# Reissuing the loads of an attention fill, moving constant rows to GpSimd, and halving ScalarE's high-part copies in a fused attention and two-MoE kernel

## The chip, the cores and the metric

The kernel runs on one NeuronCore of a Trainium2 chip. TensorE (PE, with its weight loads PEld), VectorE (DVE), ScalarE (ACT), GpSimd (POOL) and SyncE (SP) each run their own instruction stream and meet at semaphores. Times are microseconds on the device; the metric is the median over several runs.

## What is computed

A causal attention over 2 batches, 8 heads, 576 tokens and head size 64, whose scores carry a bias from a running sum; its output feeds a top-2 mixture of 8 experts, and that feeds a second mixture in which all 8 experts take every token. Everything is float32.

```python
# attention (B, H, S, D = 2, 8, 576, 64)
scores = q @ k.T / sqrt(D)
cum = cumsum(maximum(s, 0))
bias = -(cum[..., :, None] - cum[..., None, :])
scores = where(causal, -1e9, scores + minimum(bias, 0))
x = softmax(scores) @ v                      # -> (1152, 512)
# first mixture: gate with noise, the two best experts of 8
x = sum_k top2_w[k] * relu(x @ w1[e_k]) @ w2[e_k]
# second mixture: 8 rounds of row and column balancing of exp(logits), all experts
out = sum_e P[:, e] * (relu(x @ w1b[e]) @ w2b[e])
```

## The kernel before

The matmuls take float32 operands split into a high and a low part: ScalarE rounds to the high part, another engine subtracts for the low part, and PE adds the products up. The program has three stages: attention (8 heads), the sparse experts, the dense experts. The change touches the attention stage alone.

Attention works through 80 steps `k`, ten to a head (`HEAD`), five to a unit (`STEPS`, one batch of one head). Every engine has its own loop over `k` and runs parts of later steps ahead. PE does in step `k`: `rough(k + 13)` (rough scores of one query tile, for the row maximum), `turn_max` (turning two rows of maxima), `scores(k + 4)` and `mix(k)` (probabilities times values, with 65 columns a matmul). DVE does `row_max(k + 13)`, and after each unit `finish` (L1098 writes the unit's output to `x_sb`). ACT does `place_max` and `exponentials(k + 4)`, and between them the high parts of a coming head: `high_k(h)` at `k + 18 = 10 h` and `high_q(h)` at `k + 17 = 10 h`, each one copy. POOL cuts the diagonal of the probabilities (`cut`) and makes the low parts of a coming head in 8 pieces (`low_part`, from `k = 10 h - 14`; semaphore `low`).

PE waits in `rough(0)` of a head for `q_high`, `k_doubled`, `cum_loaded` and `q_rows_ready`. `scores` of a head waits for all its low pieces. `rough(k)` waits for `row_max(k - 2)`.

SP issues all loads in one order written out by hand. For a head these are `load_raw` (three transfers of 288 KB: keys, queries, keys again), `load_cum` (two rows each of the high and the low part of the running sum, put into rows 64 and 65 of `k_top`, one row of one batch at a time: four transfers of 2.25 KB), `load_v` (two transfers), `double_k` and `double_q` (the high parts copied to other partitions). Ring buffers hold 2 raw heads, 3 heads of `k_top`, `k_two`, `q_top`, `v`, and 2 heads of `q_two`. `load_raw(h)` may start when the low pieces of head `h - 2` are done:

```python
for h in range(2, H):
    sp.wait_ge(low, LOWS * (h - 1))
    load_raw(h)
    ...load_cum(h), load_v(h), double_k(h)...
    sp.wait_ge(scores_ready, HEAD * (h - Q_RING + 1))
    double_q(h)
    ...one 512 KB piece of the first expert's weights, for h = 3 to 6...
```

Before the first step PE runs `WARM_UPS` matmuls on constants (`keep_warm`, two passes each), and one half as wide between the rough steps up to `k = -5`. What stands before `k = -4`, when the first `scores` are issued, is called the fill here. In the fill, DVE clears rows 64 to 127 of the three `q_top` buffers and puts ones into rows 64 and 65 (`q_rows(w)`, two memsets each; the tiles `q_top` and `k_two` lie inside `w2l` and `w2h`, and the rows of the trace bear those names), and POOL puts ones into the same rows of `k_top`.

Of the kernel before, what the change touches and what calls it, by code (L numbers as in the profile page):

```python
# [15 lines left out]
P = 128  # L16
# [11 lines left out]
def build(nc, qT, kT, v_rows, v_tail, s, wg, wn, noise, w1, w2, gate2, w1b, w2b, out, cum_dram, x_dram, y_dram):  # L28
# [21 lines left out]
    with ExitStack() as ctx:  # L50
# [99 lines left out]
        cum_high = sem("cum_high")  # L150
        cum_low = sem("cum_low")
# [117 lines left out]
        WARM_UPS = 6  # L269
# [3 lines left out]
        K_HIGH_AHEAD, Q_HIGH_AHEAD, LOW_AHEAD = 18, 17, 14  # L273
# [48 lines left out]
        def _(sp):  # L322
            sp.dma_start(cum_s[0:G, :], s).then_inc(s_loaded, 16)

            def load_raw(h):
# [31 lines left out]
            load_cum(0)  # L357
            load_raw(1)
            double_q(0)
            load_v(0)  # L360
            load_cum(1)
            load_cum(2)
            double_k(1)
            load_v(1)
            double_q(1)
            load_v(2)
            for h in range(2, H):
                sp.wait_ge(low, LOWS * (h - 1))
                load_raw(h)
# [9 lines left out]
                double_k(h)  # L379
                sp.wait_ge(scores_ready, HEAD * (h - Q_RING + 1))  # L380
# [61 lines left out]
        def _(pool):  # L442
# [54 lines left out]
            for k in range(-LOW_AHEAD, ALL):  # L497
                if k >= 0:
# [60 lines left out]
        def _(pe):  # L559

            def rough(k):
                h, b, t = head_of(k), half_of(k), rough_tile(k)
                w, rows, width = h % HEADS_RING, rows_in(t), min(S, (t + 1) * P)
                if k % HEAD == 0:
# [280 lines left out]
        def _(act):  # L845
# [22 lines left out]
            def high_k(h):  # L868
                w = h % RAW_RING
# [4 lines left out]
                act.copy(k_two[h % HEADS_RING], k_raw[:, w, :]).then_inc(k_high, 1)  # L874

            def high_q(h):
                w = h % RAW_RING
# [563 lines left out]
```

## Time and profile before

| | us |
|---|---|
| median of 3 runs | 1310.83 |
| the three runs | 1299.89, 1310.83, 1320.83 |
| the profiled execution's own time | 1305.9 |
| its span in the trace | 1303.9 |
| PE busy | 1257.8 (96% of the span) |

PE's busy time is modelled: matmuls overlap, and a full share doesn't tell how fast they go. The granted clock (PEclk) does: 1.00 stands for 2.4 GHz and 0.50 for 1.2 GHz. Attention takes the first 169 us of the span, the sparse experts and the dense experts the rest.

### The profile page before, as it was taken

The page shows a single profiled execution, that of the slowest core. Times are in us where ns is not written, and L with a number is a line of the kernel's source. Part 1 is how long each engine was busy: PE and PEld are TensorE (multiplying, and loading weights), DVE is VectorE, ACT ScalarE, POOL GpSimd, SP SyncE. Part 2 cuts the span into 40 slices and gives each one's busy share as a digit, 9 for nine tenths or more (in the row PEclk, how much of TensorE's full clock was granted, in tenths as well). Part 3 has the DMA queues.
Part 4 walks back from the last instruction along what each step waited for, and adds up shares of the span by engine and source line. Part 5 has one row for each costly group of instructions (what it writes and reads, how often), then busy time and mean ns, then how long its engine had stood idle before and what let it go on. Part 6 is the DMA issues. An engine that isn't in the chain of part 4 may idle for free.

```text
span 1303.9 us, 17447 instructions
## 1 busy us (share of the span) xinstructions
PE 1257.8 (96%) x6607; PEld 1118.2 (86%) x6607; DVE 489.6 (38%) x1095; ACT 362.7 (28%) x682; POOL 146.5 (11%) x221
## 2 busy tenths in 40 slices
PE   7999948999999979999999999999999999999999
PEld 5888837888888857999999999999999999999997
DVE  6333457455554443344224214214214214313321
ACT  3434624344444423123113113112112112112211
POOL 5434621111110252000000000000000000000000
PEclk8556977999999979999999999999999999999999
DMA  6434253344454653001101101101101101100000
GB/s 138 107 92 116 46 205 111 125 170 171 171 175 170 202 178 129 1 1 65 65 1 64 64 0 64 64 0 64 64 0 64 64 0 64 64 0 0 24 24 24
DMA packets 24757, 102.90 MB, mean 79 GB/s; under 512 B 5440, under 2 KB 10048, under 8 KB 20752
## 3 DMA queue, kind: packets, MB, share of 16 engines
q1 hardware_dynamic: 18288, 85.89, 19.8%
q0 software_dynamic: 3360, 11.01, 2.9%
q10 hardware_dynamic: 3072, 5.51, 1.2%
q8 instruction: 22, 0.36, 0.1%
q14 instruction: 15, 0.12, 0.0%
HBM read 87.68 MB, written 10.22 MB: 75 GB/s over the span
## 4 chain that ended last, share of the span: by engine, by line
PE 90%; DVE 3%; DMA 2%; POOL 1%; SPq 1%; issue 1%; ACT 1%; DVEq 0%; POOLq 0%; ACTq 0%
PE bank L700 14%; PE bank L699 14%; PE bank L698 13%; PE bank L680 13%; PE bank L681 13%; PE bank L682 13%; PE bank L630 4%; PE bank L579 2%; PE bank L613 1%; PE bank L614 1%; DMA k_raw<-in_kT 1%; PE bank L732 1%; POOL w1l L493 1%; DMA x_sb<-x_dram,gather_at 1%; SPq L344 1%
## 5 line engine op out<-in xcount | busy, mean ns | idle before, releaser
L680 PE MATMUL bank<-xTh,w1h 128*128 128x384 f32 (+1 forms) x1024 | 343.7, 336 | 3.0 <-DVE xTl L1141 1.6
L681 PE MATMUL bank<-xTl,w1h 128*128 128x384 f32 (+1 forms) x1024 | 341.7, 334 | 0.0
L682 PE MATMUL bank<-xTh,w1l 128*128 128x384 f32 (+1 forms) x1024 | 341.2, 333 | 0.0
L937 ACT ACTIVATE hh<-bank 128x384 fp32r<-128x384 f32 (+1 forms) x256 | 123.4, 482 | 656.6 <-PE bank L682 654.8
L700 PE MATMUL bank<-w2h,hl 128*128 128x512 f32 (+1 forms) x768 | 303.6, 395 | 0.0
L699 PE MATMUL bank<-w2l,hh 128*128 128x512 f32 (+1 forms) x768 | 302.1, 393 | 0.0
L698 PE MATMUL bank<-w2h,hh 128*128 128x512 f32 (+1 forms) x768 | 301.0, 392 | 0.0
L1161 DVE SCALAR_TENSOR_TENSOR hl<-bank,hh 128x384 fp32r<-128x384 f32 (+1 forms) x256 | 139.4, 544 | 371.4 <-ACT hh L937 367.8
L680 PEld LDWEIGHTS bank<-xTh,w1h 128*128 128x128 f32 x1024 | 193.5, 189 | 5.5 <-issue 2.0
L681 PEld LDWEIGHTS bank<-xTl,w1h 128*128 128x128 f32 x1024 | 193.4, 189 | 1.2
L682 PEld LDWEIGHTS bank<-xTh,w1l 128*128 128x128 f32 x1024 | 193.3, 189 | 0.0
L699 PEld LDWEIGHTS bank<-w2l,hh 128*128 128x128 f32 (+1 forms) x768 | 142.3, 185 | 34.7
L698 PEld LDWEIGHTS bank<-w2h,hh 128*128 128x128 f32 (+1 forms) x768 | 142.5, 185 | 33.2
L700 PEld LDWEIGHTS bank<-w2h,hl 128*128 128x128 f32 (+1 forms) x768 | 142.6, 186 | 32.6
L1188 DVE SCALAR_TENSOR_TENSOR x_sb<-bank,share_now,x_sb 128x512 f32<-128x512 f32 x63 | 47.2, 750 | 259.5 <-PE bank L700 259.5
L1165 DVE TENSOR_TENSOR w2l<-raw,w2h 128x512 fp32r<-128x512 f32 x120 | 82.9, 690 | 0.0
L630 PEld LDWEIGHTS bank<-v_sb,probT 128*128 128x128 f32 (+1 forms) x480 | 74.5, 229 | 6.1 <-issue 1.2
L941 ACT CAST w2h<-raw 128x512 fp32r<-128x512 f32 x128 | 78.3, 612 | 0.0
L630 PE MATMUL bank<-v_sb,probT 128*128 128x65 f32 (+1 forms) x480 | 75.8, 310 | 0.4 <-POOL probT L487 0.4
L1079 DVE CUSTOM_DVE_ANT_0 unused<-bank,causal 64x576 fp32r<-64x576 f32 (+4 forms) x80 | 43.0, 541 | 80.0 <-PE bank L579 79.5
L1107 DVE TENSOR_TENSOR w1l<-raw,w1h 128x1024 fp32r<-128x1024 f32 x60 | 69.5, 1220 | 2.9 <-ACT w1h L916 2.9
L916 ACT CAST w1h<-raw 128x1024 fp32r<-128x1024 f32 x60 | 58.5, 1059 | 0.0
(171 smaller groups left out, 719.7 us busy)
## 6 DMA issues: line engine op xcount, KB each, us to landing
raw<-in_w SPq DMA_DIRECT2D x15, 2048.0 KB, 7.9
raw<-in_w1b SPq DMA_DIRECT2D x8, 2048.0 KB, 7.7
raw<-in_w2b SPq DMA_DIRECT2D x8, 2048.0 KB, 7.8
k_raw<-in_kT SPq DMA_DIRECT2D x16, 288.0 KB, 5.9
y_dram<-x_sb ACTq DMA_DIRECT2D x16, 256.0 KB, 3.0
q_raw<-in_qT SPq DMA_DIRECT2D x8, 288.0 KB, 5.6
q_two<-w2l SPq DMA_DIRECT2D x8, 288.0 KB, 3.2
x_dram<-x_sb SPq DMA_DIRECT2D x1, 2304.0 KB, 9.3
```

What stands on the lines that cost most here:

```text
L630: mm = pe.matmul(bank[rows, OUT_AT + n % 2, t * (HD + 1):(t + 1) * (HD + 1)], probT[:, n % UNIT_RING, at:at + nrow], v_sb[:, w, j, (HD + 1 ...
L680: pe.matmul(dst, w1h[:, c, fs], xTh[:, c, ts], start=(c == 0), stop=False)
L681: pe.matmul(dst, w1h[:, c, fs], xTl[:, c, ts], start=False, stop=False)
L682: mm = pe.matmul(dst, w1l[:, c, fs], xTh[:, c, ts], start=False, stop=(c == DC - 1))
L698: pe.matmul(dst, hh[:, f, ts], w2h[:, f, :], start=(f == 0), stop=False)
L699: pe.matmul(dst, hh[:, f, ts], w2l[:, f, :], start=False, stop=False)
L700: mm = pe.matmul(dst, hl[:, f, ts], w2h[:, f, :], start=False, stop=(f == FC - 1))
L937: act.activation(hh[:, f, 0:n_cols], bank[:, f % UP_BANKS, 0:n_cols], ACT.Relu).then_inc(st.hh_ready, 1)
L941: act.copy(w2h[:, f, :], raw2[:, f, :]).then_inc(st.w2h_ready, 1)
L1107: v.tensor_tensor(w1l[:, c, :], raw1[:, c, :], w1h[:, c, :].bitcast(F32), ALU.subtract).then_inc(st.w1_ready, 1)
L1161: v.scalar_tensor_tensor(out=hl[:, f, 0:n_cols], in0=bank[:, f % UP_BANKS, 0:n_cols], scalar=0.0, in1=hh[:, f, 0:n_cols].bitcast(F32), op0 ...
L1165: v.tensor_tensor(w2l[:, f, :], raw2[:, f, :], w2h[:, f, :].bitcast(F32), ALU.subtract).then_inc(st.w2_ready, 1)
```

## The change

- **SP's order in the fill.** The raw loads of heads 0 and 1 are issued first. Of head 0 the four rows of the running sum are then loaded one by one (batch 0 first). The high and low running sums of all heads are stored to a piece of DRAM (`cum_rows`, inside `x_dram`, which is not yet in use), and from head 1 on `load_cum` is one transfer from there. In the fill that makes 27 transfers instead of 31 (the raw load of head 2 counted in both), and one instead of four for each later head's sums.
- **SP's order in the loop.** `load_raw(h + 1)` comes right behind `double_k(h)`, ahead of the wait of `double_q(h)` and of the weights' piece.
- **Waits of PE.** `rough(0)` waits for batch 0's two rows alone (`cum_first`); batch 1's are waited for five steps later.
- **Constant rows.** POOL clears and sets the rows of `q_top` as well as those of `k_top` (`constant_rows`): those of buffers 0 and 1 at the start, those of buffer 2 behind the low pieces of head 0. DVE no longer does.
- **High parts.** ScalarE's copies are made in halves of 576 columns (1024 columns of the weights in halves of 512), one half behind each of four successive `exponentials`, from `k + 19 = 10 h`.
- **Warm-ups.** 8 instead of 6.

```diff
-        WARM_UPS = 6
+        WARM_UPS = 8
...
-        K_HIGH_AHEAD, Q_HIGH_AHEAD, LOW_AHEAD = 18, 17, 14
+        HIGH_AHEAD, LOW_AHEAD = 19, 14
...
         def high_at(k):
-            kh, qh = divmod(k + K_HIGH_AHEAD, HEAD), divmod(k + Q_HIGH_AHEAD, HEAD)
-            return (kh[0] if kh[1] == 0 else None, qh[0] if qh[1] == 0 else None)
+            h, part = divmod(k + HIGH_AHEAD, HEAD)
+            return (h, *divmod(part, 2)) if h > 1 and part < 4 else None
...
+            cum_rows = x_dram[0:2 * H * N // DM].rearrange("a (c d) -> (a c) d", d=P).rearrange("(g x) d -> g (x d)", g=G).rearrange(
+                "g (r s) -> g r s", r=2)
...
             def load_cum(h):
                 w = h % HEADS_RING
                 if h < HEADS_RING:
                     sp.wait_ge(aug_ready, 2 + h)
-                for row, part, ready in ((HD, cum_h, cum_high), (HD + 1, cum_l, cum_low)):
-                    if h == 0:
-                        sp.wait_ge(ready, 1)
-                    for b in range(B):
-                        sp.dma_start(k_top[w][row:row + 1, b * S:(b + 1) * S].bitcast(F32),
-                                     part[h * B + b:h * B + b + 1, :].bitcast(F32)).then_inc(cum_loaded[w], 16)
+                if h == 1:
+                    sp.wait_ge(cum_stored, 32)
+                sp.dma_start(k_top[w][HD:HD + 2, :].rearrange("r (b s) -> r b s", b=B).bitcast(F32),
+                             cum_rows[h * B:(h + 1) * B].rearrange("b r s -> r b s")).then_inc(cum_loaded[w], 16)
...
             load_raw(0)
-            load_cum(0)
             load_raw(1)
+            sp.wait_ge(aug_ready, 2)
+            sp.wait_ge(cum_high, 1)
+            first_cum(HD, cum_h, 0, cum_first)
+            sp.wait_ge(cum_low, 1)
+            first_cum(HD + 1, cum_l, 0, cum_first)
+            first_cum(HD, cum_h, 1, cum_loaded[0])
+            first_cum(HD + 1, cum_l, 1, cum_loaded[0])
             double_q(0)
+            sp.dma_start(cum_rows[:, 0, :], cum_h[0:G, :].bitcast(F32)).then_inc(cum_stored, 16)
+            sp.dma_start(cum_rows[:, 1, :], cum_l[0:G, :].bitcast(F32)).then_inc(cum_stored, 16)
+            double_k(1)
+            load_cum(1)
             load_v(0)
-            load_cum(1)
+            sp.wait_ge(low, LOWS)
+            load_raw(2)
+            double_q(1)
             load_cum(2)
-            double_k(1)
             load_v(1)
-            double_q(1)
             load_v(2)
             for h in range(2, H):
-                sp.wait_ge(low, LOWS * (h - 1))
-                load_raw(h)
...
                 double_k(h)
+                if h + 1 < H:
+                    sp.wait_ge(low, LOWS * h)
+                    load_raw(h + 1)
                 sp.wait_ge(scores_ready, HEAD * (h - Q_RING + 1))
                 double_q(h)
...
-            for w in range(HEADS_RING):
+            def constant_rows(w):
                 pool.memset(k_top[w][HD:P, :].bitcast(F32), 1.0).then_inc(aug_ready, 1)
-            pool.wait_ge(aug_ready, HEADS_RING + 1)
+                pool.memset(q_top[w][HD:P, :].bitcast(F32), 0.0).then_inc(q_rows_clear, 1)
+                pool.wait_ge(q_rows_clear, w + 1)
+                pool.memset(q_top[w][HD:HD + 2, :].bitcast(F32), 1.0).then_inc(q_rows_ready, 1)
+            constant_rows(0)
+            constant_rows(1)
...
             for k in range(-LOW_AHEAD, ALL):
+                if k == LOWS - LOW_AHEAD:
+                    pool.wait_ge(low, LOWS)
+                    constant_rows(2)
+                    pool.wait_ge(q_rows_ready, 3)
...
-                    pe.wait_ge(cum_loaded[w], 64 * (h // HEADS_RING) + 64)
+                    if h == 0:
+                        pe.wait_ge(cum_first, 32)
+                if h == 0 and k == STEPS:
+                    pe.wait_ge(cum_loaded[0], 32)
+                elif h and k % HEAD == 0:
+                    pe.wait_ge(cum_loaded[w], 16 * (h // HEADS_RING + (1 if w else 2)))
...
-                act.copy(k_two[h % HEADS_RING], k_raw[:, w, :]).then_inc(k_high, 1)
+                part = act.copy(k_two[h % HEADS_RING][:, cols], k_raw[:, w, cols])
+                if half:
+                    part.then_inc(k_high, 1)
```

On SP, from the first load of the running sum to the raw load of head 2 (`k_raw` and `q_raw` from `in_kT` and `in_qT` are raw loads; `w2l` and `w2h` as sources are the high parts), before:

```order
L344 DMA k_top<-cum_h 1x16x36 [waits cum_high,aug_ready]
...
L333 DMA v_sb<-in_v_rows 128x4x128
L334 DMA v_sb<-in_v_tail 64x128
L344 DMA k_top<-cum_h 1x16x36 [waits aug_ready]
...
L350 DMA k_top<-w2h 64x1152 [waits k_high]
L333 DMA v_sb<-in_v_rows 128x4x128
L334 DMA v_sb<-in_v_tail 64x128
L354 DMA q_two<-w2l 64x1152 [waits q_high]
L333 DMA v_sb<-in_v_rows 128x4x128
L334 DMA v_sb<-in_v_tail 64x128
L327 DMA k_raw<-in_kT 64x1152 [waits low]
```

and now:

```order
L351 DMA k_top<-cum_h 1x16x36 [waits cum_high,aug_ready]
...
L360 DMA q_two<-w2l 64x1152 [waits q_high]
L372 DMA x_dram<-cum_h 16x576
L373 DMA x_dram<-cum_l 16x576
L356 DMA k_top<-w2h 64x1152 [waits k_high]
L347 DMA k_top<-x_dram 2x2x576 [waits cum_stored,aug_ready]
L338 DMA v_sb<-in_v_rows 128x4x128
L339 DMA v_sb<-in_v_tail 64x128
L332 DMA k_raw<-in_kT 64x1152 [waits low]
```

The raw load of head 2 was the 29th transfer of the queue and is the 19th.

On DVE, from its first instruction to the first row maximum (`L1079`, now `L1111`), before:

```order
L1052 MEMSET zeros_g 16x576
L1048 MEMSET w2l 64x1152
L1050 MEMSET w2l 2x1152
L1055 TENSOR_SCALAR cum_p<-cum_s 16x576
L1056 SCALAR_TENSOR_TENSOR cum_s<-cum_p,zeros_g 16x576
L1058 CAST k_top<-k_raw 64x1152
L1060 TENSOR_TENSOR cum_l<-cum_s,cum_h 16x576
L1048 MEMSET w2l 64x1152
...
L1048 MEMSET w2l 64x1152
L1050 MEMSET w2l 2x1152
L1067 COPY rinv<-ones 128x10
L1079 ISA unused,aug<-bank,causal 64x576
```

and now:

```order
L1087 MEMSET zeros_g 16x576
L1088 MEMSET probT 64x2x64
L1089 MEMSET v_sb 64x3x128
L1091 TENSOR_SCALAR cum_p<-cum_s 16x576
L1092 SCALAR_TENSOR_TENSOR cum_s<-cum_p,zeros_g 16x576
L1094 CAST k_top<-k_raw 64x1152
L1096 TENSOR_TENSOR cum_l<-cum_s,cum_h 16x576
L1099 COPY rinv<-ones 128x10
L1111 ISA unused,aug<-bank,causal 64x576
```

The six memsets of `q_top` (under the name `w2l`) are gone from DVE's queue.

On ACT, around the high parts of head 2, before:

```order
L866 CAST w2l<-bank 2x192 [waits max_turned]
L855 ACTIVATE probT<-bank 128x512 [waits scores_ready]
L874 CAST w2h<-k_raw 128x1152 [waits k_again0,k_loaded0]
L855 ACTIVATE probT<-bank 128x448 [waits scores_ready]
L881 CAST w2l<-q_raw 64x1152 [waits q_loaded0]
```

and now:

```order
L900 CAST w2l<-bank 2x192 [waits max_turned]
L889 ACTIVATE probT<-bank 128x512 [waits scores_ready]
L908 CAST w2h<-k_raw 128x576 [waits k_again0,k_loaded0]
L889 ACTIVATE probT<-bank 128x448 [waits scores_ready]
L908 CAST w2h<-k_raw 128x576 [waits k_again0,k_loaded0]
L889 ACTIVATE probT<-bank 128x320 [waits scores_ready]
L917 CAST w2l<-q_raw 64x576 [waits q_loaded0]
```

The wait for the raw keys stands behind the same exponential as before; the second half of the keys and the queries stand one exponential further back.

## Rows read from the trace of the kernel before

**Rows 1.** Windows: busy us of each engine, then PEclk, DMA share, GB/s.

```profile
14.00:15.00 1.00, 0.00 (x0) 0.00 (x0) 0.93 (x3) 0.00 (x0) 0.92 (x2) 0.97 0.98 221
21.00:22.00 1.00, 1.00 (x5) 0.83 (x3) 0.32 (x3) 0.00 (x0) 1.00 (x2) 0.62 0.72 152
35.00:36.00 1.00, 1.00 (x9) 0.78 (x9) 0.90 (x6) 0.84 (x4) 0.46 (x1) 0.71 0.47 97
40.00:60.00 20.00, 20.00 (x95) 17.70 (x96) 6.61 (x28) 6.99 (x17) 6.08 (x13) 0.50 0.23 54
120.00:121.00 1.00, 1.00 (x7) 0.96 (x7) 0.24 (x2) 0.61 (x2) 0.00 (x1) 0.63 0.00 0
```

**Rows 2.** Timeline, 25 to 34 us: start, duration, instruction, idle before and its releaser.

```profile
25.82 0.60 SPq L329 DMA_DIRECT2D k_raw<-in_kT  x1
...
31.84 1.15 ACT L874 CAST w2h<-k_raw 128x1152 fp32r<-128x1152 f32 x1 [2.95 <-DMA k_raw<-in_kT]
...
33.49 0.36 PE L613 MATMUL bank<-w2l,k_top 128*128 128x192 f32 x1 [1.64 <-ACT probT L855]
```

**Rows 3.** Line L1098 on DVE, once in each unit: start and duration.

```profile
35.85 0.42 DVE L1098 TENSOR_TENSOR x_sb<-bank,rinv 128x256 f32<-128x256 f32 x1
...
116.64 0.42 DVE L1098 TENSOR_TENSOR x_sb<-bank,rinv 128x256 f32<-128x256 f32 x1
125.20 0.42 DVE L1098 TENSOR_TENSOR x_sb<-bank,rinv 128x256 f32<-128x256 f32 x1
131.68 0.42 DVE L1098 TENSOR_TENSOR x_sb<-bank,rinv 128x256 f32<-128x256 f32 x1
138.94 0.42 DVE L1098 TENSOR_TENSOR x_sb<-bank,rinv 128x256 f32<-128x256 f32 x1
145.55 0.42 DVE L1098 TENSOR_TENSOR x_sb<-bank,rinv 128x256 f32<-128x256 f32 x1
```

**Rows 4.** Timeline of the fill, 0 to 24 us.

```profile
2.42 8.23 PE L636 MATMUL bank<-causal,ones 128*128 128x512 f32 x12 [2.42 <-POOL causal L452]
2.42 3.05 POOL L456 MEMSET k_top<- 64x1152 f32 x3
...
7.20 0.67 ACT L890 CAST cum_h<-cum_s 16x576 fp32r<-16x576 f32 x1 [4.75 <-DVE cum_s L1056]
...
9.07 3.04 POOL L477 TENSOR_TENSOR q_two<-q_raw,w2l 64x288 fp32r<-64x288 f32 x4 [3.60 <-ACT w2l L881]
...
9.20 0.19 PEld L636 LDWEIGHTS bank<-causal,ones 128*128 128x128 f32 x1 [0.24 <-issue]
...
9.63 0.19 PEld L636 LDWEIGHTS bank<-causal,ones 128*128 128x128 f32 x1 [0.24 <-issue]
...
11.84 0.45 PE L579 MATMUL bank<-k_top,w2l 96*64 96x512 f32 x2 [1.20 <-DMA k_top<-cum_l]
...
12.25 3.39 POOL L477 TENSOR_TENSOR w2h<-k_raw,w2h 64x288 fp32r<-64x288 f32 x4
...
13.33 1.02 DVE L1050 MEMSET w2l<- 2x1152 f32 x1 [0.30 <-PE bank L579]
...
15.65 0.69 PE L579 MATMUL bank<-k_top,w2l 96*128 96x384 f32 x1 [2.19 <-DVE aug L1079]
...
21.87 0.53 PE L579 MATMUL bank<-k_top,w2l 96*128 96x384 f32 x1
...
23.92 0.50 PE L613 MATMUL bank<-w2l,k_top 128*128 128x512 f32 x1
```

**Rows 5.** Timeline around the raw load of head 7, 127 to 137 us.

```profile
127.27 0.60 SPq L329 DMA_DIRECT2D k_raw<-in_kT  x1
...
136.57 0.36 PE L613 MATMUL bank<-w2l,k_top 128*128 128x192 f32 x1 [0.83 <-ACT probT L855]
```

**Rows 6.** DMA issues of the whole run: count, KB each, median us to landing.

```profile
k_raw<-in_kT SPq DMA_DIRECT2D x16, 288.0 KB, 5.9
...
y_dram<-x_sb ACTq DMA_DIRECT2D x8, 160.0 KB, 2.0
```

More of the change, by code:

```diff
@@ L150, in build @@
         cum_high = sem("cum_high")
+        cum_first = sem("cum_first")
+        cum_stored = sem("cum_stored")
         cum_low = sem("cum_low")
@@ L339, in load_cum, with first_cum @@
                     sp.wait_ge(aug_ready, 2 + h)
-                for row, part, ready in ((HD, cum_h, cum_high), (HD + 1, cum_l, cum_low)):
-                    if h == 0:
-                        sp.wait_ge(ready, 1)
-                    for b in range(B):
-                        sp.dma_start(k_top[w][row:row + 1, b * S:(b + 1) * S].bitcast(F32),
-                                     part[h * B + b:h * B + b + 1, :].bitcast(F32)).then_inc(cum_loaded[w], 16)
+                if h == 1:
+                    sp.wait_ge(cum_stored, 32)
+                sp.dma_start(k_top[w][HD:HD + 2, :].rearrange("r (b s) -> r b s", b=B).bitcast(F32),
+                             cum_rows[h * B:(h + 1) * B].rearrange("b r s -> r b s")).then_inc(cum_loaded[w], 16)
+            def first_cum(row, part, b, done):
+                sp.dma_start(k_top[0][row:row + 1, b * S:(b + 1) * S].bitcast(F32), part[b:b + 1, :].bitcast(F32)).then_inc(done, 16)
             def double_k(h):
@@ L866, in place_max, with high_k @@
                 act.copy(q_top[w][ROWS_ROUGH:ROWS_ROUGH + 2, b * S + i0:b * S + i1], bank[0:2, MAX_AT, 0:i1 - i0]).then_inc(max_placed, 1)
-            def high_k(h):
-                w = h % RAW_RING
+            def high_k(h, half):
+                w, cols = h % RAW_RING, slice(half * S, (half + 1) * S)
                 act.wait_ge(k_loaded[w], 16 * (h // RAW_RING) + 16)
@@ L873, in high_k, with high_q @@
                     act.wait_ge(scores_ready, HEAD * (h - HEADS_RING + 1))
-                act.copy(k_two[h % HEADS_RING], k_raw[:, w, :]).then_inc(k_high, 1)
-            def high_q(h):
-                w = h % RAW_RING
+                part = act.copy(k_two[h % HEADS_RING][:, cols], k_raw[:, w, cols])
+                if half:
+                    part.then_inc(k_high, 1)
+            def high_q(h, half):
+                w, cols = h % RAW_RING, slice(half * S, (half + 1) * S)
                 act.wait_ge(q_loaded[w], 16 * (h // RAW_RING) + 16)
@@ L880, in high_q, with high_w1 @@
                     act.wait_ge(scores_ready, HEAD * (h - HEADS_RING + 1))
-                act.copy(q_top[h % HEADS_RING][0:HD, :], q_raw[:, w, :]).then_inc(q_high, 1)
-            def high_w1(c):
+                part = act.copy(q_top[h % HEADS_RING][0:HD, cols], q_raw[:, w, cols])
+                if half:
+                    part.then_inc(q_high, 1)
+            def high_w1(c, half):
+                cols = slice(half * F // 2, (half + 1) * F // 2)
                 act.wait_ge(first_w1[c] if c < DC - 1 else SP_.raw1_loaded, 16)
-                act.copy(w1h[:, c, :], raw1[:, c, :]).then_inc(SP_.w1h_ready, 1)
+                part = act.copy(w1h[:, c, cols], raw1[:, c, cols])
+                if half:
+                    part.then_inc(SP_.w1h_ready, 1)
             act.wait_ge(const_ready, 5)
@@ L890, in _ @@
             act.copy(cum_h[0:G, :], cum_s[0:G, :]).then_inc(cum_high, 1)
-            high_q(0)
-            high_k(0)
-            high_k(1)
-            high_q(1)
-            for k in range(-ROUGH_AHEAD, ALL):
-                kh, qh = high_at(k)
-                if kh is not None and kh > 1:
-                    if kh < H:
-                        high_k(kh)
-                    else:
-                        high_w1(2 * (kh - H))
-                if qh is not None and qh > 1:
-                    if qh < H:
-                        high_q(qh)
-                    else:
-                        high_w1(2 * (qh - H) + 1)
+            for h in range(2):
+                for half in range(B):
+                    high_q(h, half)
+                for half in range(B):
+                    high_k(h, half)
+            for k in range(-ROUGH_AHEAD, ALL):
                 for n, part in turns_at(k):
@@ L911, in _ @@
                     exponentials(k + SCORES_AHEAD)
+                high = high_at(k)
+                if high is not None:
+                    h, of, half = high
+                    if h >= H:
+                        high_w1(2 * (h - H) + of, half)
+                    elif of == 0:
+                        high_k(h, half)
+                    else:
+                        high_q(h, half)
             def split_w1(st, n):
```

13 lines of the change are left out of this document (4 added, 9 removed).

## The prediction, as it was put on record

> **What bounds the kernel now.** I read the stretches with their granted clock first, then the timeline where that clock changes, then the period of a unit. Over the whole run PE is the bound, so in attention, too, the question is what PE waits for and how fast it goes. The second is the larger one. In the stretch from 40 to 60 us PE is busy for 20.00 of 20 us, yet its clock is granted at 0.50, that is 1.2 GHz [rows 1]. The clock has fallen inside the slice from 35 to 36 us (mean 0.71) and is back inside the one from 120 to 121 us (mean 0.63) [rows 1]: 85 us of attention run at the lower level. What PE did just before it fell stands in the timeline: it stood still for 1.64 us up to 33.49, waiting for an exponential, and ScalarE was late with that because its high-part copy of head 2 had waited 2.95 us for the raw keys, whose last transfer SP had issued only at 25.82 [rows 2]. The same pair, a stop and a fall, stands in the fill: 2.19 us of idle up to 15.65 [rows 4], the fall at the end of the slice from 14 to 15, the return inside the slice from 21 to 22 [rows 1]. Shorter stops didn't bring it down: 1.20 us up to 11.84 [rows 4] and 0.83 us up to 136.57 [rows 5].
>
> What the clock costs is read from DVE's one instruction per unit. Seven units between 35.85 and 116.64 took 80.8 us, 11.54 each; after the return, the two without a stall took 6.48 and 6.61, mean 6.55 [rows 3].
>
> **The fill.** PE's two added warm-ups are four passes. At the pace that the last passes had (9.20 to 9.63, 0.43 us), they add 1.7 us to the end at 10.65, so PE reaches `rough(0)` at 12.4; before, it started at 11.84, when the running sum's rows landed [rows 4]. They should now land earlier: DVE starts the sum's chain behind fewer memsets, and two rows instead of four are waited for. They queue behind head 1's raw loads, however. So the warm-ups set the start, at a cost of 0.5 us. The next wait goes away. PE idled from 13.46 to 15.65 for DVE's first row maximum, which stood behind two pairs of memsets of 1.02 us each (the last at 13.33) [rows 4]; they leave DVE's queue. `rough(2)` then follows 1.6 us behind `rough(0)`, as 13.46 does on 11.84: at 14.0 instead of 15.65, a gain of 1.65. From there to the first scores there were five rough steps in 6.2 us, most of them at the low clock, and three in 2.05 us at the high one (21.87 to 23.92) [rows 4], so 1.24 us a step against 0.68. At the high clock DVE's row maxima begin to hold PE, so I take 0.95, the middle; five steps gain 1.45. The fill gains **3.1 us** (between 1.2, if the clock still falls, and 4.4, if 0.68 holds for all), and the first scores start at 20.8 instead of 23.92.
>
> What GpSimd takes over is 2 memsets more per buffer, 1.02 us each by its own three (3.05) [rows 4]. Those of the first two buffers end about 9 us, and it waited for `q_high` until 9.07 in any case [rows 4]; those of the third start behind head 0's low pieces, which end at 15.64, and delay head 1's low pieces by 3.1 us at most. The first reader of these is `scores(10)`, ten steps behind the first scores, past 30 us: nothing. Without that cover it would be 3.1 us. The new wait of SP is the one for `cum_stored`. The two stores are issued at about 10 us; the nearest prices are 2.0 us for a store of 160 KB and 5.9 us for a load in a full queue [rows 6], so it ends between 12 and 16 us. Behind it stand the sum's rows and the values of head 0 and the raw load of head 2, and this last waits for the low pieces until 15.64 anyway. Nothing, or 0.5 us at worst.
>
> **The stall of head 2.** Its raw load was the 29th transfer of SP and is the 19th. It can be issued at 15.7, its last transfer at 17.5, and lands 5.9 us later [rows 6], at 23.4. ScalarE wants it behind the same exponential as before. That was 28.89 (31.84 less 2.95), 5.0 us after the first scores, so now 25.8: 2.4 us to spare. The idle **1.6 us** goes, and with it what preceded the fall of the clock.
>
> **The clock.** If it stays at 2.4 GHz, seven units of 11.54 become seven of 6.55, 34.9 us less, and the unit in which it rose (116.64 to 125.20, 8.56) gives 2.0: **36.9 us**. It needs later raw loads in time at the faster pace. The one load that the trace shows at that pace, of head 7, came too late: the unit took 7.26 instead of 6.55 [rows 3], PE idle 0.83 [rows 5]. In the new order a raw load is released two steps earlier (2.6 us at 1.31 a step) and goes ahead of a 512 KB weight piece instead of behind it. Against a stop of 0.83 that is cover enough, and it gives **0.7 us**.
>
> The Trainium skill speaks against this term. Its page "TensorE: Matmul & The Clock Gate", section "A second HAM failure mode: psum-queue depth-cycling", tells of a kernel in which frequent short idle spells between groups of matmuls swung the clock between its levels, with no long wait. By that the slow stretch wouldn't hang on the stall, and the sum would keep 3.1 + 1.6 + 0.7 alone: 1300 (rival 1), instead of the 1264 below. The two falls in this trace each followed a stop of 1.64 us or more, which speaks for the rows.
>
> **ScalarE's halves.** A copy of 1152 columns took 1.15 us [rows 2]; for 576 the nearest row is 0.67 (the running sum's) [rows 4], so four halves cost 2.7 instead of 2.3 per head, 3 us over all heads. ScalarE was busy for 6.99 of 20 us at the low clock, which is 0.62 of the time at the fast pace (6.99 / 20 x 11.54 / 6.55), and a half delays the next exponential less than a whole copy did: nothing. The loads of the running sum, 15 fewer in the loop, shorten SP's queue, which has waits of its own there.
>
> **Sum.** 3.1 + 1.6 + 36.9 + 0.7 = 42.3 us off the profiled execution's 1305.9: **1264**. That execution lies 4.9 below the median of 1310.83; the three runs spread over 21 us, about four units' worth of the difference between the two clocks (5.0 us a unit), so I take the spread to be the length of the slow stretch, and expect the changed kernel to spread less. A measurement here tells about 2% from no change: the forecast is 3.6% below the median.
>
> **Rivals.** (1) *The clock falls without a long stop.* The stream of attention itself, matmuls of 65 columns with small gaps, could pull it down again somewhere. For it speaks that 80 us of this stream didn't bring the clock back, and that its return at 120 us has no visible cause; against it, that the clock held from 22 to 35 us and from 121 us on under the same stream. If it falls soon and for as long as before, only 3.1 + 1.6 + 0.7 remain: 1300; if half as long, 1282. (2) *The reissue doesn't do what it says.* Something else, the store to DRAM or the low pieces, holds head 2's raw load past 25.8, and the stop and the fall stay: 1305.9 less 3.1 and 0.7, 1302. It needs 2.4 us more than I count. (3) *Slower.* Head 1's raw loads now stand ahead of the first sum rows in the queue. If those land so late that PE stops for as long as it did at 13.46 (2.19 us brought the clock down, 1.20 did not [rows 4]), that is past about 14 us, the clock falls before the first scores, and if the warm matmuls don't bring it back it stays low for all of attention. Then the eight units that ran fast cost up to 11.54 less 6.8 each (mean of the three measured), 38 us, and 1305.9 + 38, less 1.2 + 1.6 + 0.7, gives 1340.
>
> **Chances and range.** Forecast 0.75, with its own range of 1257 to 1271 (the fill's bounds, and a few us of run to run). Rival 1: 0.13, spread over 1275 to 1302; rival 2: 0.07; rival 3: 0.05. The range that leaves out 2 in 10 reaches from 1256 into the first rival, to 1292. More than 2% faster is below 1284.6: the forecast and less than half of rival 1, 0.80. Within 2%: the rest of it, rival 2 and some of rival 3, 0.16. Slower: 0.04.
>
> **What the changed profile should show.** A granted clock of 1.00 from the low twenties to past 160 us; DVE's line of a unit every 6.5 to 6.7 us, the first at about 31; PE's first `rough` at 12.4 behind the last warm-up; no PE idle behind an exponential that waited for raw keys; SP issuing head 2's raw load at about 16. The prediction is wrong if a stretch at 0.50 stays, however short the stops; or if the units at the high clock take clearly more than 6.6 us, another engine being the bound.

## The result, and the profile after

The changed kernel took **1262.88 us** (median of 4: 1258.55, 1261.05, 1264.71, 1305.5) against 1308.61 for the kernel before (median of 4), a ratio of 0.966, interval 0.9585 to 0.9737: 3.4% faster. The forecast was 1264. The execution of 1305.5, whose mean granted clock was 0.944 where the others had 0.978 to 0.984, is left out of the ratio, as the longest executions of a kernel are in every ratio below. The profiled execution took 1261.05 us, its span 1259.3; before, the span was 1303.9, so there are 44.6 us to account for.

The stretches with their granted clock (PEclk is the third number from the end), the counterpart of [rows 1]:

```profile
14.00:15.00 1.00, 1.00 (x7) 0.83 (x6) 0.95 (x6) 0.00 (x0) 0.92 (x2) 1.00 1.03 212
21.00:22.00 1.00, 1.00 (x11) 0.92 (x9) 1.00 (x5) 0.95 (x3) 1.00 (x3) 1.00 1.04 230
35.00:36.00 1.00, 1.00 (x14) 0.93 (x13) 0.20 (x2) 0.60 (x2) 0.78 (x3) 1.00 0.00 0
40.00:60.00 20.00, 19.76 (x167) 17.59 (x166) 11.21 (x47) 12.70 (x31) 13.14 (x27) 1.00 0.81 192
120.00:121.00 1.00, 0.84 (x8) 0.60 (x7) 0.41 (x1) 0.31 (x1) 1.00 (x3) 1.00 0.00 0
```

The clock is 1.00 in all of them. PE is busy for 19.76 of 20 us between 40 and 60 (20.00 before), yet ran 167 matmuls there instead of 95: the busy share alone doesn't tell the two kernels apart. (Behind attention, where PE waits for the gates, the clock falls in both, at about 182 before and 135 now; that part is unchanged.)

DVE's one instruction per unit, the counterpart of [rows 3] (it stands at L1130 now):

```profile
30.58 0.42 DVE L1130 TENSOR_TENSOR x_sb<-bank,rinv 128x256 f32<-128x256 f32 x1
37.06 0.42 DVE L1130 TENSOR_TENSOR x_sb<-bank,rinv 128x256 f32<-128x256 f32 x1
...
75.56 0.42 DVE L1130 TENSOR_TENSOR x_sb<-bank,rinv 128x256 f32<-128x256 f32 x1
81.78 0.42 DVE L1130 TENSOR_TENSOR x_sb<-bank,rinv 128x256 f32<-128x256 f32 x1
...
100.95 0.42 DVE L1130 TENSOR_TENSOR x_sb<-bank,rinv 128x256 f32<-128x256 f32 x1
...
124.23 0.42 DVE L1130 TENSOR_TENSOR x_sb<-bank,rinv 128x256 f32<-128x256 f32 x1
```

Set beside the same units of before, they share the 44.6 us out. The first unit ends 5.3 earlier (30.58 for 35.85). The next seven take 44.98 (30.58 to 75.56) for 80.8: 35.8. The eighth takes 6.22 for 8.56: 2.3. The three after it take 19.17 (81.78 to 100.95) for 20.35: 1.2. From there to the end nothing changes.

The fill, and the loads behind it, in the timeline of the changed kernel (start, duration; in brackets the engine's idle time and who ended it), beside [rows 2] and [rows 4]:

```profile
2.42 8.65 PE L670 MATMUL bank<-causal,ones 128*128 128x512 f32 x16 [2.42 <-POOL causal L469]
5.19 3.33 DVE L1094 CAST k_top<-k_raw 64x1152 fp32r<-64x1152 f32 x1
5.85 1.05 POOL L474 MEMSET k_top<- 64x1152 f32 x1
7.96 1.55 POOL L477 MEMSET w2l<- 2x1152 f32 x1
9.20 0.53 SPq L351 DMA_DIRECT2D k_top<-cum_l  x1
12.07 0.45 PE L613 MATMUL bank<-k_top,w2l 96*64 96x512 f32 x2 [0.99 <-DMA k_top<-cum_l]
13.48 0.44 PE L613 MATMUL bank<-k_top,w2l 96*128 96x384 f32 x1
16.33 1.05 POOL L474 MEMSET k_top<- 64x1152 f32 x1
16.57 0.60 SPq L332 DMA_DIRECT2D k_raw<-in_kT  x1
17.85 0.60 SPq L334 DMA_DIRECT2D k_raw<-in_kT  x1
18.44 1.05 POOL L477 MEMSET w2l<- 2x1152 f32 x1
18.92 0.50 PE L647 MATMUL bank<-w2l,k_top 128*128 128x512 f32 x1
19.57 3.08 POOL L502 TENSOR_TENSOR q_two<-q_raw,w2l 64x288 fp32r<-64x288 f32 x4
22.60 0.30 POOL L512 TENSOR_SCALAR_AFFINE_SELECT probT<-probT 128x128 f32<-128x128 f32 x1
22.95 0.43 PE L664 MATMUL bank<-v_sb,probT 128*128 128x65 f32 x2 [0.87 <-POOL probT L512]
24.87 0.67 ACT L908 CAST w2h<-k_raw 128x576 fp32r<-128x576 f32 x1
```

The 2.19 us stop of the fill is gone, and so is the one of 1.64 us behind ScalarE: head 2's raw load is issued from 16.57 on, and its high part (24.87) waits for nothing. In their place stands one stop that wasn't there before: `mix(0)`, at 22.95, waited 0.87 us for GpSimd. GpSimd made the third buffer's constant rows (16.33 to 19.49), then head 1's four query low pieces (19.57 to 22.65), and only then cut the diagonal that `mix(0)` reads. The weight loads of the next two `mix` wait for the cut as well:

```profile
24.29 0.52 PEld L664 LDWEIGHTS bank<-v_sb,probT 128*128 128x128 f32 x4 [0.38 <-POOL probT L512]
25.60 0.74 PEld L664 LDWEIGHTS bank<-v_sb,probT 128*128 128x128 f32 x6 [0.27 <-POOL probT L512]
```

These two are waits of PEld, not idle time of PE, which the trace has busy with its last matmuls there. What all three cost together is read from the run below that has the rows of `q_top` on DVE and none of these waits: from the first scores to the first unit's end it takes 10.08 us, the changed kernel 11.66, so 1.6 us.

### The profile page after: what moved, and what is told of

Its sections match the earlier page's. It is cut to its first block, busy times and chain, and to the rows that moved or that the text cites. A ratio compares the mean times of both kernels' runs of the same rounds, so it can differ in the third digit from the quotient of the medians.

```text
span 1259.3 us, 17471 instructions
## 1 busy us (share of the span) xinstructions
PE 1216.9 (97%) x6611; PEld 1082.8 (86%) x6611; DVE 486.3 (39%) x1089; ACT 365.0 (29%) x702; POOL 153.7 (12%) x227
## 4 chain that ended last, share of the span: by engine, by line
PE 92%; POOL 2%; DVE 2%; DMA 1%; ACT 1%; issue 1%; POOLq 0%; DVEq 0%
PE bank L734 14%; PE bank L733 14%; PE bank L732 14%; PE bank L714 14%; PE bank L715 14%; PE bank L716 14%; PE bank L664 3%; PE bank L613 1%; PE bank L647 1%; PE bank L648 1%; PE bank L766 1%; POOL w1l L518 1%; DMA x_sb<-x_dram,gather_at 1%; POOL q_two L502 0%; PE bank L678 0%
## 5 line engine op out<-in xcount | busy, mean ns | idle before, releaser
L664 PEld LDWEIGHTS bank<-v_sb,probT 128*128 128x128 f32 (+1 forms) x480 | 53.8, 173 | 5.9 <-POOL probT L512 2.7
L1111 DVE CUSTOM_DVE_ANT_0 unused<-bank,causal 64x576 fp32r<-64x576 f32 (+4 forms) x80 | 42.8, 541 | 40.8 <-PE bank L613 40.5
L664 PE MATMUL bank<-v_sb,probT 128*128 128x65 f32 (+1 forms) x480 | 57.2, 255 | 1.3 <-POOL probT L512 1.3
```

Source lines behind the costliest of these rows:

```text
L664: mm = pe.matmul(bank[rows, OUT_AT + n % 2, t * (HD + 1):(t + 1) * (HD + 1)], probT[:, n % UNIT_RING, at:at + nrow], v_sb[:, w, j, (HD + 1 ...
```

## The experiments

Those on the kernel before ask which edit keeps the clock up; those on the changed kernel, which of its edits are needed. They ran in three sessions, in which the kernel before had medians of 1311.49 (the early load alone, the late load, the filled stop, the loop undone), 1315.34 (both orders, the rows by DVE, whole copies, the version without the stop) and 1311.02 (the rest). How long the clock is down differs between executions of one kernel, so a median of few moves with it, and the ends are given too. Each run left one trace, that of one execution.

**Head 2's raw load alone, on the kernel before.**

```diff
             double_k(1)
+            sp.wait_ge(low, LOWS)
+            load_raw(2)
             load_v(1)
...
             for h in range(2, H):
-                sp.wait_ge(low, LOWS * (h - 1))
-                load_raw(h)
+                if h > 2:
+                    sp.wait_ge(low, LOWS * (h - 1))
+                    load_raw(h)
```

> The kernel before, with one edit: the raw load of head 2 is issued ahead of the values of head 1 instead of behind those of head 2, five transfers earlier. Theory (the stop of PE at head 2 brings the clock down): PE no longer idles 1.64 us there, the clock holds after the fill, seven units go from 11.5 to about 6.5 us; the loop's loads are as late as before, so some 0.7 us per head stay: 1266 to 1274 us. Rival A (the clock falls in attention by itself): only the stop goes, about 1303. Rival B (what the fill did to the clock, or DVE's memsets, is what counts): the clock falls all the same, about 1303.

Measured: 1311.92 (median of 4, 1266.91 to 1318.64): no gain in the median. One of the four, 1266.91 at a mean clock of 0.981, lies in the expected range; the other three had 0.933 to 0.942. The trace (1307.51) shows why. PE's timeline first, then the stretches with their clock:

```profile
57.71 0.36 PE L616 MATMUL bank<-w2l,k_top 128*128 128x192 f32 x1 [1.25 <-ACT probT L858]
...
71.70 0.36 PE L616 MATMUL bank<-w2l,k_top 128*128 128x192 f32 x1 [0.96 <-ACT probT L858]
```

```profile
70.00:75.00 5.00, 4.04 (x34) 3.23 (x32) 2.07 (x11) 4.28 (x9) 1.54 (x4) 0.94 0.37 78
75.00:80.00 5.00, 5.00 (x23) 4.61 (x21) 1.46 (x4) 1.58 (x3) 4.60 (x9) 0.50 1.00 252
```

Head 2's stop and the fall behind it are gone. But at the faster pace the loop's later raw loads come late: ScalarE waited 2.55 and 2.26 us for raw keys, PE stood still for 1.25 and 0.96, and the clock fell behind the second of these, for the rest of attention. The early load alone is not enough to keep the clock up in most executions.

**The loop's order alone, on the kernel before.** `load_raw(2)` stays at the end of the fill; the loop is the changed one.

```diff
             load_v(2)
+            sp.wait_ge(low, LOWS)
+            load_raw(2)
             for h in range(2, H):
-                sp.wait_ge(low, LOWS * (h - 1))
-                load_raw(h)
...
                 double_k(h)
+                if h + 1 < H:
+                    sp.wait_ge(low, LOWS * h)
+                    load_raw(h + 1)
```

> The kernel before with the loop's part of SP's order alone: each raw load from head 3 on right behind the copy of the keys; head 2's raw load stays at the end of the fill. Theory (a late raw load at any head brings the clock down): PE stops about 1.6 us at head 2 and the clock falls there in most executions, 1295 to 1315 us. Rival (the loop's loads alone were the matter): 1264 to 1268 in most.

Measured: 1295.05 (median of 4, 1278.03 to 1318.96). The stop of head 2 is still there, and the fall with it; the first line is ScalarE's wait ahead of it:

```profile
31.61 1.15 ACT L877 CAST w2h<-k_raw 128x1152 fp32r<-128x1152 f32 x1 [2.92 <-DMA k_raw<-in_kT]
...
33.26 0.36 PE L616 MATMUL bank<-w2l,k_top 128*128 128x192 f32 x1 [1.62 <-ACT probT L858]
```

```profile
36.00:84.00 48.00, 48.00 (x220) 42.35 (x219) 15.11 (x64) 16.91 (x38) 19.53 (x41) 0.50 0.46 108
```

The clock was granted at 0.82 from 33 to 36, at 0.50 from there to 84, and was back inside the stretch from 84 to 87.

**Both orders, nothing else, on the kernel before.** The two diffs above together: neither the stored sums, nor the constant rows, nor the halves, nor the warm-ups.

> The kernel before with SP's order alone: head 2's raw load five transfers earlier in the fill, and in the loop each raw load right behind the copy of the keys. The running sums still go row by row, DVE still clears rows, ScalarE still copies whole heads. Theory (late raw loads, at head 2 and then at each head at the fast pace, are what brings the clock down): no stop of PE behind raw keys anywhere, 1305.9 less 1.6, 36.9 and 0.7: 1264 to 1270 us in most executions, the fill as before. Rival (the shorter queue, GpSimd's rows or the halves are needed for it): stops stay and the clock falls, 1295 to 1318.

Measured: **1264.54** (median of 4, 1262.07 to 1264.73), 0.961 of that session's median of the kernel before; beside the quicker of that kernel's executions alone the ratio is 0.977 (0.9709 to 0.9837). The stretch of attention that ran at 0.50 before:

```profile
40.00:60.00 20.00, 20.00 (x167) 17.69 (x166) 12.10 (x53) 13.29 (x31) 12.80 (x27) 1.00 0.74 175
```

The fill is as before (its 2.19 us stop ends at 15.67, and the clock is low from 15 to 22), the first unit ends at 34.10 instead of 30.58, and from there on a unit takes 6.2 to 6.5 us. SP's order in two places is worth all of the change but some 2 to 4 us (1264.54 for 1262.88 by the medians, 3.1 by the unit that ends at 104.03 here and at 100.95 in the changed kernel).

**The loop's order undone, on the changed kernel.**

```diff
             for h in range(2, H):
+                if h > 2:
+                    sp.wait_ge(low, LOWS * (h - 1))
+                    load_raw(h)
...
-                if h + 1 < H:
-                    sp.wait_ge(low, LOWS * h)
-                    load_raw(h + 1)
```

> The changed kernel, with one edit: in the loop, the raw loads of heads 3 to 7 go back to where they were (behind the queries' copy and the weights' piece). Theory: each comes up to 1 us late at the fast pace, stops too short for the clock, 5 x 0.7 us: 1265 to 1268 us, the clock at 1.00. Rival (short stops also bring the clock down): 1280 to 1305.

Measured: 1298.01 (median of 4, 1276.59 to 1303.65). A stop of 0.65 at 54.42 left the clock up, this one did not; the clock fell inside the stretch from 70 to 75 and stayed at 0.50 to the end of attention:

```profile
69.43 0.35 PE L647 MATMUL bank<-w2l,k_top 128*128 128x192 f32 x1 [1.56 <-ACT probT L889]
```

The prediction gave the loop's order 0.7 us. It is worth some 35, since without it the clock is lost later.

**Head 2's raw load late again, on the changed kernel.** `load_raw(2)` with its wait stands behind `load_v(2)`.

```diff
-            sp.wait_ge(low, LOWS)
-            load_raw(2)
             double_q(1)
...
             load_v(2)
+            sp.wait_ge(low, LOWS)
+            load_raw(2)
```

> The changed kernel, with one edit: the raw load of head 2 goes back to the end of the fill, behind the values of head 2. It is then issued near 22 us, lands near 29, and ScalarE wants it at 24.9, so PE stops for 2 to 4 us. Theory: the clock falls behind this stop and stays down for most of attention, 1298 to 1310 us. Rivals A and B (the stop does not matter to the clock): 1263 plus the stop alone, 1265 to 1268.

Measured: 1262.87 (median of 4; three at 1260.16 to 1262.91, one at 1291.38), as the changed kernel. ScalarE and PE in the timeline:

```profile
27.54 0.67 ACT L908 CAST w2h<-k_raw 128x576 fp32r<-128x576 f32 x1 [2.57 <-DMA k_raw<-in_kT]
...
28.71 0.36 PE L647 MATMUL bank<-w2l,k_top 128*128 128x192 f32 x1 [0.32 <-ACT probT L889]
```

The expected stop didn't come. With the shorter queue the load was issued at 20.53 instead of the 24.26 with the loop's order alone, but ScalarE also wanted it earlier, and waited 2.57 us for it, nearly the 2.92 of that run. PE had 0.32 us left to wait instead of 1.62. Of these 1.3 us, 0.35 is the shorter wait of ScalarE, 0.48 that only half a copy stands ahead of the exponential (0.67 us for 1.15), and the rest that PE finished the work ahead of the stop later. So the early place isn't needed once all other edits are there; which of these others is enough beside the loop's order, no run shows.

**The stop of head 2 filled with work, on the kernel before.** Five idle-time matmuls on constants, 256 columns each, ahead of `scores(8)`; the load is as late as before.

```diff
+                if k == 4:
+                    for _ in range(5):
+                        keep_warm(BANK // 2)
```

> The kernel before, with one edit: ahead of the scores that wait in the stop at head 2, PE runs five 256-column matmuls on constants (some 2.2 us), so that it is busy in the stop instead of idle; the load is as late as before. Theory, if PE's standing still is what brings the clock down: the wait stays, the clock does not fall, 1268 to 1278 us. Rival A (the clock falls by itself), or if late data and not idleness is behind it: 1304 to 1308.

Measured: 1302.6 (median of 11, 1271.79 to 1320.08), 9 us below that session's median of the kernel before, and not the 1268 to 1278 expected; 3 of the 11 lie below 1290, where the lowest of the session's 13 executions of the kernel before was 1298.03. The trace (1320.08) has PE busy for 35.61 of the 36 us from 24 to 60, at a clock of 1.00: with the late data still late, but PE kept at work until they are there, there is no fall at 35.

```profile
24.00:60.00 36.00, 35.61 (x280) 31.32 (x279) 19.55 (x78) 20.94 (x48) 22.59 (x46) 1.00 0.69 157
```

The fall comes behind the next stop instead:

```profile
60.40 0.35 PE L613 MATMUL bank<-w2l,k_top 128*128 128x192 f32 x1 [0.80 <-ACT probT L858]
```

```profile
60.00:65.00 5.00, 4.60 (x31) 3.86 (x32) 1.55 (x11) 3.64 (x9) 2.84 (x6) 0.81 0.60 124
65.00:70.00 5.00, 5.00 (x21) 4.62 (x22) 1.46 (x4) 0.98 (x2) 4.38 (x9) 0.50 0.99 250
```

So the fall at 35 goes with PE's standing still and not with the late transfer: the two traces of the kernel before and the loop alone, with the stop, have it, and this one, the early load alone and both orders, without the stop, don't.

**The rows of `q_top` by DVE again, on the changed kernel** (`q_rows(0)`, `(1)`, `(2)` where they were; GpSimd sets the rows of `k_top` alone).

```diff
-            constant_rows(0)
-            constant_rows(1)
...
-                    constant_rows(2)
...
+            q_rows(0)
             v.wait_ge(s_loaded, 16)
```

> The changed kernel with the constant rows of the query buffers back on DVE, at the places they had. Theory: a fill matter only, PE waits some 2 us for the first row maximum, the clock falls near 15 us and is back before the first scores or soon behind: 3 to 5 us more than the changed kernel, 1264 to 1268. Rival (the fill's fall is what carries on into attention): 1295 to 1315.

Measured: 1262.89 (median of 4, 1261.69 to 1263.0), the changed kernel's time and not the 3 to 5 us more that were expected. A stop in the fill is back (1.78 us up to 15.76; the clock stayed up behind it), and the first scores start at 21.22 instead of 18.92; but `mix(0)` no longer waits, and the first unit ends at 31.30 against 30.58. Of 2.3 us gained at the first scores, 0.7 are left one unit later.

**Whole copies on ScalarE, on the changed kernel** (`high_k`, `high_q`, `high_w1` as one copy each, one behind each of two exponentials).

```diff
-            return (h, *divmod(part, 2)) if h > 1 and part < 4 else None
+            return (h, part) if h > 1 and part < 2 else None
```

> The changed kernel with ScalarE's high parts copied whole, keys and queries behind two successive exponentials (the places of the kernel before). Theory: hidden, 1260 to 1265 us. Rival (a whole copy makes an exponential late often enough for the clock): 1280 to 1305.

Measured: 1260.05 (median of 4, 1259.18 to 1264.85): with the load early the halves are worth nothing. The stop at `mix(0)` took 1.09 us here, and the clock fell behind it (the stretches with their clock):

```profile
24.00:26.00 2.00, 2.00 (x9) 1.53 (x9) 0.00 (x0) 1.25 (x3) 1.63 (x4) 0.50 1.19 226
...
27.00:28.00 1.00, 1.00 (x8) 0.96 (x8) 0.00 (x0) 1.00 (x2) 0.92 (x2) 0.93 0.58 120
```

It was back after some 3 us, so the time hardly shows it.

**Six warm-ups, on the changed kernel.**

```diff
-        WARM_UPS = 8
+        WARM_UPS = 6
```

> The changed kernel with 6 warm-ups instead of 8. Theory: PE idles up to 1.7 us longer ahead of the first rough scores, whose data land at 12.07 in any case; the clock may fall in the fill, for 0 to 4 us: 1261 to 1267. Rival (the two more warm-ups keep the clock for attention): 1285 or more in most executions.

Measured: 1268.78 (median of 4: 1259.17, 1260.73, 1276.84, 1295.56). Two of the four lie above the expected 1261 to 1267. The lower two are the changed kernel's time: PE waits for the sum's rows up to 11.95 in any case. The trace is of the highest, and there the clock fell inside the stretch from 24 to 27, behind 0.95 us of idle at `mix(0)`, and came back inside 105 to 108.

**The changed kernel again**, for more executions.

> The changed kernel once more, to count how often a slow stretch comes. Theory: 1258 to 1265 us in at least 3 of 4 executions, the others 1285 to 1306.

Measured: 1258.32, 1258.33, 1259.83, 1264.37, 1277.37, 1295.6, 1318.6. Four of seven are within the expected 1258 to 1265, where at least three in four were; with the first four, 4 of 11 executions lie above 1277. The trace is of the one at 1295.6, PE's timeline and then the stretches:

```profile
22.95 0.44 PE L664 MATMUL bank<-v_sb,probT 128*128 128x65 f32 x2 [0.73 <-POOL probT L512]
```

```profile
24.00:27.00 3.00, 3.00 (x17) 2.36 (x15) 0.76 (x2) 2.17 (x5) 2.41 (x5) 0.71 0.83 178
...
40.00:60.00 20.00, 20.00 (x95) 17.50 (x95) 6.14 (x27) 7.51 (x19) 6.42 (x14) 0.50 0.44 103
105.00:108.00 3.00, 3.00 (x16) 2.66 (x16) 0.76 (x2) 0.89 (x2) 2.75 (x6) 0.64 0.57 182
```

The only stop over half a microsecond between 15 and 100 us is the one at `mix(0)`, the stop that the change itself brought, 0.73 us here; the clock fell some 2.3 us after its end and stayed low for about 80 us.

**A version without that stop.** On the changed kernel, GpSimd makes the third buffer's `k_top` rows at the start and its `q_top` rows behind `cut(4)` and `cut(5)`; DVE makes `cum_l` ahead of the cast of `k_top`; the small loads of the gates stand behind `double_q(4)`; the splitting of the gates is spread over six steps; and SP waits for that cast before it loads head 2's raw data.

```diff
-                if k == LOWS - LOW_AHEAD:
-                    pool.wait_ge(low, LOWS)
-                    constant_rows(2)
-                    pool.wait_ge(q_rows_ready, 3)
                 if k >= 0:
                     cut(k)
+                if k == 4:
+                    pool.wait_ge(causal_done, k + 1)
+                    pool.memset(q_top[2][HD:P, :].bitcast(F32), 0.0).then_inc(q_rows_clear, 1)
...
-                if k == GATES_AT:
-                    split_gates()
+                if 0 <= k - GATES_AT < 6:
+                    split_gates(k - GATES_AT)
```

> The changed kernel without the stops that its trace still shows: DVE makes the low running sum ahead of the copy of the keys (0.99 us), GpSimd sets the third buffer's rows at the start and behind the cuts of steps 4 and 5 instead of between the low pieces of heads 0 and 1 (0.87, 0.38 and 0.27 us), the gates' small loads go behind the raw load of head 5 and not ahead of it (0.5 us), and DVE's gate split is spread over six steps (0.65 us). Theory: 3 us less than the changed kernel, 1257 to 1261, and the slow stretch in fewer executions than 1 in 4. Rival (the stops that are left were hidden, and the falls come whatever PE does): 1260 to 1264, slow in as many.

Measured: 1258.32 (median of 4, 1257.11 to 1261.36; ratio 0.972, 0.9656 to 0.9786, to the kernel before). The same kernel, run again for more executions:

> The version without the stops that were left once more, beside the changed kernel. Theory: 2 to 4 us less than the changed kernel's fast executions, 1257 to 1261, and slow in none or fewer.

Measured: **1257.59** (median of 6, 1256.58 to 1259.14; ratio 0.969, 0.9629 to 0.9751). All ten executions lie below 1262. In its timeline, the sum's rows and PE's first use of them:

```profile
6.68 0.53 SPq L351 DMA_DIRECT2D k_top<-cum_l  x1
...
12.64 0.45 PE L619 MATMUL bank<-k_top,w2l 96*64 96x512 f32 x2 [0.44 <-DMA k_top<-cum_l]
```

`mix(0)` no longer waits, the first unit ends at 29.61, and the clock is 1.00 through attention:

```profile
20.00:120.00 100.00, 99.49 (x829) 88.76 (x827) 54.70 (x223) 65.38 (x159) 73.59 (x143) 1.00 0.56 132
```

In the same session the changed kernel's four quickest executions have a median of 1259.1, so 1.5 us are gained there, less than the 2 to 4 expected; the larger gain is that none of ten executions lost the clock, against 4 of 11. The fill's start gained nothing: `cum_l` was issued 2.5 us earlier than in the changed kernel, and the first `rough` started 0.6 later.

## Why the prediction was right, step by step

**The clock: right, and the cause is shown.** 36.9 us were predicted and 38.1 measured (35.8 + 2.3). The chain *late raw keys, PE idle, clock down* holds: filling the idle time removed the fall at its place; undoing the loop's order on the changed kernel, or doing one of the two orders alone on the kernel before, left a stop and a fall at the place where the keys were late; and both orders alone on the kernel before kept the clock up. Undoing the early load on the changed kernel did not bring the fall back; there PE stood still for 0.32 us only.

**A wrong step inside it** was the reading that shorter stops "didn't bring it down". In attention, stops of 0.73 (changed kernel again), 0.80 (filled stop), 0.95 (six warm-ups), 0.96 (early load alone) and 1.09 (whole copies) were each followed by a fall within 3 us. Others of 0.80 (late load on the changed kernel), 0.83 [rows 5], 0.87 (the changed kernel's profile) and 1.25 (early load alone, at 57.71) were not. In the fill of the kernel before, the fall near 14.9 came while PE still stood (13.46 to 15.65), not behind the stop. All three of 1.56 to 1.64 in attention were followed by one; of those at 0.65 or 0.70, none. Nor is length all that counts: in the fill, stops of 1.55 us (the last version's first trace, up to 12.67) and 1.78 (the rows by DVE) were followed by no fall, and the one of 1.27 or 1.28 us with which attention ends, in all eleven traces that reach it at the upper level, by none for 9 us. So a stop here has a chance of costing tens of microseconds, not a fixed price. The expected smaller spread didn't come either: the changed kernel's executions reach from 1258 to 1319, and the sign that the prediction named for its being wrong, a stretch at 0.50 that stays however short the stops, is there in the changed kernel's second trace. The prediction counted stops by their own length, and so gave the loop's order 0.7 us (1.2 measured in the changed kernel) where its absence costs some 35.

**The fill: mechanism right, size off.** 3.1 us were predicted, 5.0 came (18.92 for 23.92). The eight rough steps from `rough(2)` to the first scores took 5.44 us (13.48 to 18.92), 0.68 each, the pace of the last three before; the prediction took 0.95 for five of them, in the belief that DVE's maxima would hold PE. The start was right by time (12.07, predicted 12.4) and wrong by cause: PE waited 0.99 us for the sum's rows and not for the warm-ups, which ended at 11.07. The rows, which were to land earlier, landed at 11.93 instead of 11.59: DVE did start the sum's chain earlier, but then spent 3.33 us on the cast of `k_top` where it had spent 0.72, so `cum_l` was issued at 9.20, and the rows came in right behind head 1's raw loads (the last of them landed at 11.60).

**The constant rows: the step that failed.** "Nothing", since the first reader of the third buffer comes past 30 us. The rows themselves are read late, but GpSimd works in order, and behind them and head 1's low pieces stood `cut(0)`, which `mix(0)` reads at 22. This cost 1.6 us (11.66 against the 10.08 of the run with these rows by DVE), so that the 1.6 us of head 2's stop, which did go, are left as 0.3 between the first scores and the first unit's end (11.66 for 11.93). Worse, this stop is of the kind that can bring the clock down: in the one execution of the changed kernel above 1277 that has a trace, the fall came behind it. That the others have the same cause wasn't seen, but the counts speak for it: of the four kernels with this stop (the changed one, the late load, whole copies, six warm-ups) 7 of 23 executions lie above 1275, of the three without it that keep SP's new order (both orders, the rows by DVE, the last version) none of 18 (the last version has other edits too; the rows by DVE, 4 executions, differ in little else).

**The stall of head 2, SP's new wait, ScalarE's halves.** Head 2's load was issued from 16.57 (predicted about 16), and no wait for raw keys of head 2 or a later head is left. SP waited 1.2 us for `cum_stored`; the low pieces that head 2's load waits for in any case ended at 16.27, so this cost it 0.3 at most. Whole copies gave the same time.

**The sum.** 42.3 us were predicted and 44.6 came, but term by term it is 5.0, 0.3, 38.1 and 1.2 for 3.1, 1.6, 36.9 and 0.7. That the fill's surplus of 1.9 and the 1.3 lost behind the constant rows nearly cancel is luck, and so, with 4 of 11 executions above 1277, is in part that only one of the first four was.

**The rivals.** Rival 1, a fall without a stop, was not seen: each fall in the traces of attention stands behind a stop of 0.73 us or more. Its page of the Trainium skill ("TensorE: Matmul & The Clock Gate", "A second HAM failure mode: psum-queue depth-cycling") speaks of short idle spells; the runs agree in that stops under 1 us were followed by falls, but a stream without one (the last version) held its clock through all of attention. Rival 2 was wrong. Of rival 3 the queueing is real: in the last version a row issued at 6.68 landed at 12.51, behind the raw loads, and was used at 12.64. It is too short to reach the 14 us from which that rival decided.

**What stays open** is when the clock comes back, and why it falls behind one stop of 0.80 us and not behind another. The low stretches lasted 3 us (whole copies), about 50 (the loop alone), 80 (the changed kernel again, six warm-ups) and 85 (before), all with PE busy, and with the early load alone, the loop undone and the filled stop they lasted to the end of attention. Where the clock came back inside attention, nothing that I found in the trace marks it.

## What to carry to other kernels

Price a stop of TensorE by what it can do to the clock behind it, and not by its length: here one of 0.73 us stood ahead of a loss of 37 (1295.6 against 1258). When a transfer is made punctual and the kernel speeds up, the next one must be punctual at the new pace, or the gain is lost a few units later; so undo and do each part alone before crediting it. And before calling a moved instruction free, list what is queued behind it on its own engine, not only who reads its result.

## What the runs showed of the hardware

- **A busy TensorE can stay at 1.2 GHz.** In the profile of before, 85 us at 0.50 with PE busy throughout [rows 1]. The Trainium skill ("TensorE: Matmul & The Clock Gate", "What's actually happening") says that the throttled level is the default and that activity releases it; here the same stream of matmuls held 2.4 GHz when it had it, and didn't win it back for 80 us and more.
- **A cast on VectorE takes longer beside GpSimd's memsets.** The cast of 64 x 1152 float32 values took 0.72 us on DVE with GpSimd idle (before, and with the rows of `q_top` by DVE), 3.33 beside GpSimd's memsets in the changed kernel and 1.93 in the last version; one of these memsets took 1.55 us instead of 1.05. Not every instruction is slowed: DVE's scan just ahead of the cast took 1.35 us both with GpSimd idle (before) and beside the memsets. Before:

```profile
7.09 0.72 DVE L1058 CAST k_top<-k_raw 64x1152 fp32r<-64x1152 f32 x1
```

  The Trainium skill ("GPSIMD Engine Reference", "1. Specifications") says that GpSimd shares its SBUF interfaces with VectorE and names contention with some DVE instructions; the rows agree. The run with the rows by DVE had the same raw loads in flight beside the cast, so these aren't the cause; no run took the memsets away alone.
- **An early issue need not be an early landing.** Behind six raw loads of 288 KB, `cum_l` issued at 9.20 landed at 11.93, and issued at 6.68 at 12.51; the last raw load landed at 11.60 and 11.83. Before, behind three raw loads that had landed by 7.39, it was issued at 9.23 and landed at 10.93. So the moment of issue didn't decide.
